# Other orders of work in an attention, Strassen feed-forward and Fourier kernel on one core

## The chip, the core and the metric

The kernel runs on one core of one Trainium2 chip. The metric is the device time of one execution in microseconds (us), as the median of several runs. A profile of one further execution stands beside them. Engines are called by the names of the profile: PE (TensorE, its weight loads apart as PEld), DVE (VectorE), ACT (ScalarE), POOL (GpSimd, called Pool in the text) and SP, which only issues transfers.

## The reference, cut to what matters

```python
x = windowed_attention(q, k, v)            # 2 batches, 8 heads, 768 x 64, ALiBi bias, 96 local keys and 8 global ones
x = x.transpose(0, 2, 1, 3).reshape(2, 768, 512)
u = x + (x.transpose(0, 2, 1) @ U @ V).transpose(0, 2, 1)        # rank 32
x = u + np.maximum(u @ w_ch1, 0) @ w_ch2                         # 512 -> 2048 -> 512
u = x + np.real(fft(fft(x, axis=1), axis=2))
un = (u - mean(u)) / np.sqrt(var(u) + 1e-6)
out = u + np.maximum(un @ moe2_w_ch1, 0) @ moe2_w_ch2
```

All is fp32. The kernel gets near full precision from PE by splitting each factor into a high part and the rest (names with H and L), and by three matmuls per product: high by high, high by low, low by high.

## The kernel before, in words

**Stages.** The attention is 48 steps of two query tiles each, run as slots 0 to 50 (a slot does the scores of its step, the transposes of the step two before, and the products with V of the step three before). Slots 0 to 32 (FFN_SLOT = 33) come first. Then come 32 rounds of the feed-forward part: rounds 0 to 7 are batch 0 of the first layer, 8 to 15 batch 1, 16 to 23 and 24 to 31 the second layer. The remaining 18 attention slots, the 22 mixing pieces of batch 1 (the rank 32 product), the splits of the next batch's factors and the Fourier steps are put between the items of the rounds.

**A round.** It makes 256 of the 2048 hidden columns, and adds their share of the output. The first product of the layer is done by the Winograd form of Strassen's scheme, in seven block products P1 to P7 (`product`, lines 706 to 735, six matmuls of 384 columns each). ITEMS (line 51) is the order of a round: P1, P5, L0, P6, L1, P2, L2, L3, P7, L4, L5, P3, P4. L0 to L5 are the six output tiles of the round before (`out_tile`, lines 737 to 756, six matmuls of 512 columns each). A gap is the place behind an item; gap number 13 g + i stands behind item i of round g, and `put` fills it (FILL, lines 314 to 317). All engines go through the items and gaps in the same order, each with its own part, in order.

**Banks.** P1 and P2 gather in Xb, P5 and P3 in Zb, P6, P7 and P4 in Yb. ACT copies P1 and P5 out (P1s, P5s), DVE adds P1s to Yb (L1262, item P6), ACT copies that back to P1s (L976), DVE adds it to Zb (L1266, item L1) and P5s to Yb into Xb (L1272, item P7). Four halves of the hidden block come from this; for each ACT does the relu (hidH, L962) and DVE the rest (hidL, L1242): relu(0, 0) at item P2, relu(1, 1) at P7, where it first waits until all tiles of the round before are made, relu(0, 1) at P3, relu(1, 0) at P4. The semaphore s_hidl counts the four. Each output tile takes one of two banks yP, and can start only when DVE has added the tile two before it to Y (L1249).

**Weights.** SP loads the first layer's blocks of a round two rounds ahead (w_load), and the output weights one round ahead (o_load). For round g + 1, ACT makes the high parts WCH in round g (`w_hi`, L952, part 0 at item L0 and part 1 at item L1; part 1 waits for the sums), and Pool the low parts WCL (`w_lo`, L518, four instructions). WOH is ACT's (L959, item L3), WOL Pool's (`o_lo`, L524, two instructions). `w_sums` (L507 to L512, Pool) makes the four sums of the weight blocks, two rounds ahead.

**The other factor.** RAW holds the transposed input of a batch, TT its four sums T1 to T4, made by `u_sums` on Pool (L542 to L548, 8 instructions over k = 0 to 3). UCH and UCL are the split factors. For batch 0 they are made in the attention (`first_split`, slots 15, 21, 27 and 32). For the others `split(c, name)` makes each of the seven in the gap 2, 4, 6, 7, 10, 13 or 15 places behind the start of the round before the change: ACT casts (L930) when the product that last used the old one is made, DVE subtracts (L1228). At the first, ACT waits for all the sums of that batch. CHANGES is 8, 16, 24. Pool's order in its loop (lines 550 to 575): w_lo(g + 1), o_lo(g), w_sums(g + 2), u_sums for a change at g + 2, then in rounds 7 and 8 the tables of the Fourier matrices, split into high and low (CSH, CSL: 2310 columns; CDH, CDL: 1028 columns). Ahead of the loop it is w_sums(0), w_lo(0), w_sums(1), u_sums(0, k).

**Fourier steps.** `fourier_slots` places them from round 8 (b + 1) + 1 on, for batch b. On DVE: fold (3 parts, twice), split, edge, seq, mid, and for each of three pairs of tiles dim (PE alone), combine (adds the transform to Y, then bn_stats and bn_aggr, L1346 to L1364), norm (L1374) and turn (PE transposes, ACT writes RAW, L1044). The first fold waits for CSL and CDL. Steps stand every 2.5 gaps per slot, at any item.

Of the kernel before, what the change touches and what calls it, by code (L numbers as in the profile page):

```python
# [22 lines left out]
ALU = mybir.AluOpType  # L23
# [27 lines left out]
ITEMS = ("P1", "P5", "L0", "P6", "L1", "P2", "L2", "L3", "P7", "L4", "L5", "P3", "P4")  # L51
PRODUCTS = ("P1", "P5", "P6", "P2", "P7", "P3", "P4")
# [45 lines left out]
def program(nc, q_t, k_t, v, k_win, v_win, n_local, n_global, moe_U, moe_V, w_in, w_out,  # L98
            seq_dft, dim_dft, ident_in, out):
    ctx = ExitStack()  # L100
    with ctx:
# [202 lines left out]
        FFN_SLOT = 33  # L304
# [31 lines left out]
        def split_slot(slot):  # L336

            return (slot - 15) // 6 if slot in (15, 21, 27) else KD - 1 if slot == FFN_SLOT - 1 else None
# [6 lines left out]
        for c, g in enumerate(CHANGES):  # L345
            for product, late in zip(PRODUCTS, (2, 4, 6, 7, 10, 13, 15)):
                put(GAPS * (g - 1) + late, "split", c, product)
# [25 lines left out]
        def fourier_slots(b):  # L373
            at = GAPS * (FPAIRS * (b + 1) + 1)

            def later(slot, *what):
                put(at + int(2.5 * slot), "fourier", b, *what)

            for slot, *what in ((0, "fold", 0, 0), (0.4, "fold", 0, 1), (0.8, "fold", 0, 2), (1.2, "split", 0), (2, "edge"), (4, "seq", 0, 0),
                                (4.4, "fold", 1, 0), (4.8, "fold", 1, 1), (5.2, "seq", 0, 1), (5.2, "fold", 1, 2), (7, "split", 1),  # L380
                                (9, "seq", 1, 0), (10, "seq", 1, 1), (11, "seq", 2, 0), (12, "mid")):
                later(slot, *what)
            order = []
            for i, slot in enumerate((13, 18, 22)):
                for part in range(2):
                    order.append((slot + part, 0, "dim", i, part))
                    for late, what in enumerate(("combine", "norm", "turn")):
                        order.append((16 + 4 * i + 2 * late + part, 1, what, i, part))
            for slot, _, *what in sorted(order, key=lambda o: o[:2]):
                later(slot, *what)  # L390
# [9 lines left out]
        def _(sp):  # L400
# [63 lines left out]
            for g in range(ROUNDS):  # L464
# [11 lines left out]
                if g == FPAIRS:  # L476
                    sp.wait_ge(s_csplit, 1)
# [13 lines left out]
        def _(pool):  # L491
# [60 lines left out]
            w_sums(1)  # L552
            for k in range(KD):
                u_sums(0, k)
            for g in range(ROUNDS):
# [3 lines left out]
                if g + 2 < ROUNDS:  # L559
                    w_sums(g + 2)  # L560
                if g + 2 in CHANGES:
                    for k in range(KD):
                        u_sums(CHANGES.index(g + 2) + 1, k)
# [900 lines left out]
```

## Time and profile before

| what | us |
|---|---|
| runs | 742.34, 742.73, 746.5 (median 742.73) |
| profiled execution | 743.1 |
| its span, first to last instruction | 741.3 |
| PE busy | 682.5 (92%), 3672 matmuls |
| PEld / DVE / ACT / POOL busy | 605.1 / 421.2 / 308.4 / 377.6 |
| mean granted clock of PE | 0.98 of full speed |

Busy time is that of one engine; engines overlap, so only the idle time of the engine that bounds a stage tells what can be won there. Idle time behind an item in brackets, as [2.65 <-DVE Y L1249], is the time the engine stood before this instruction, and what it waited for. Round g is counted from its first matmul of P1 to the next round's.

### The profile page before, as it was taken

What the parts mean: (1) busy time and instruction counts of PE and PEld (TensorE: products, weight loads), DVE (VectorE), ACT (ScalarE), POOL (GpSimd) and SP (SyncE); (2) the same over time, 40 slices, a digit from 0 to 9 for tenths busy, and PEclk for the clock granted to TensorE, in tenths of its full rate; (3) what the DMA queues carried; (4) which work ended last, traced back from release to release, by engine and by line L of the source; (5) the groups of instructions that cost most, each with busy time, mean ns of one, the idle gap of its engine ahead of it and who ended that gap; (6) DMA issues with size and microseconds to landing.
All of it is one profiled execution on the core that took longest, in us unless ns stands there. A gap on an engine that the chain in (4) does not pass through costs nothing.

```text
span 741.3 us, 10239 instructions
## 1 busy us (share of the span) xinstructions
PE 682.5 (92%) x3672; PEld 605.1 (82%) x3672; DVE 421.2 (57%) x903; ACT 308.4 (42%) x665; POOL 377.6 (51%) x365
## 2 busy tenths in 40 slices
PE   8949989999999988799997979999897889999997
PEld 6949889888898877688886869787786778899886
DVE  7526665544445386764675466653865485454544
ACT  4636676442433353234332444332343364334430
POOL 0140143244355899553453796555444876665621
PEclk9988999999999989999999999999999999999999
DMA  8332224012112313111110111111111022121132
GB/s 240 132 124 97 98 97 143 15 55 79 38 56 81 108 58 93 57 43 43 58 57 29 58 57 57 57 57 57 31 56 56 30 70 73 62 81 57 57 114 86
DMA packets 50532, 54.07 MB, mean 73 GB/s; under 512 B 4432, under 2 KB 37328, under 8 KB 50352
## 3 DMA queue, kind: packets, MB, share of 16 engines
q1 hardware_dynamic: 50480, 53.40, 22.9%
q8 instruction: 30, 0.49, 0.3%
q14 instruction: 22, 0.18, 0.1%
HBM read 53.39 MB, written 3.15 MB: 76 GB/s over the span
## 4 chain that ended last, share of the span: by engine, by line
PE 67%; DVE 12%; POOL 8%; ACT 6%; issue 5%; DMA 1%; DVEq 0%; SPq 0%; POOLq 0%; ACTq 0%
PE yP L753 10%; PE yP L755 9%; PE yP L754 9%; PE Yb L732 3%; PE Yb L733 3%; PE Yb L734 3%; PE aP L647 3%; PE aP L621 3%; PE Zb L732 2%; PE Zb L734 2%; PE Zb L733 2%; DVE Y L1249 2%; PE Xb L732 2%; PE Xb L733 2%; PE Xb L734 2%
## 5 line engine op out<-in xcount | busy, mean ns | idle before, releaser
L518 POOL TENSOR_TENSOR WCL<-w_stage,WCH 128x512 fp32r<-128x512 f32 (+1 forms) x128 | 154.7, 1230 | 204.9 <-ACT WCH L952 204.9
L1249 DVE TENSOR_TENSOR Y<-yP,Y 128x512 f32<-128x512 f32 x192 | 129.7, 684 | 89.4 <-PE yP L755 89.1
L753 PE MATMUL yP<-WOH,hidH 128*128 128x512 f32 x384 | 155.6, 405 | 24.6 <-DVE Y L1249 22.8
L755 PE MATMUL yP<-WOH,hidL 128*128 128x512 f32 x384 | 153.1, 399 | 0.0
L754 PE MATMUL yP<-WOL,hidH 128*128 128x512 f32 x384 | 152.6, 397 | 0.0
L524 POOL TENSOR_TENSOR WOL<-o_stage,WOH 128x512 fp32r<-128x512 f32 x64 | 86.0, 1366 | 46.6 <-ACT WOH L959 46.6
L753 PEld LDWEIGHTS yP<-WOH,hidH 128*128 128x128 f32 x384 | 73.5, 191 | 43.7 <-DVE Y L1249 28.2
L962 ACT ACTIVATE hidH<-Xb 128x384 fp32r<-128x384 f32 x64 | 31.4, 491 | 182.1 <-PE yP L755 174.3
L1242 DVE SCALAR_TENSOR_TENSOR hidL<-Xb,hidH 128x384 fp32r<-128x384 f32 x64 | 35.6, 556 | 89.8 <-ACT hidH L962 89.8
L755 PEld LDWEIGHTS yP<-WOH,hidL 128*128 128x128 f32 x384 | 73.0, 190 | 16.2
L754 PEld LDWEIGHTS yP<-WOL,hidH 128*128 128x128 f32 x384 | 73.3, 191 | 11.0
L732 PE MATMUL Yb<-UCH,WCH 128*128 128x384 f32 x192 | 66.5, 346 | 1.6 <-DVE UCL L1222 1.6
L733 PE MATMUL Yb<-UCL,WCH 128*128 128x384 f32 x192 | 65.5, 341 | 0.0
L734 PE MATMUL Yb<-UCH,WCL 128*128 128x384 f32 x192 | 65.4, 341 | 0.0
L952 ACT CAST WCH<-w_stage 128x768 fp32r<-128x768 f32 x64 | 60.2, 943 | 0.9 <-DMA w_stage<-w_in 0.9
L882 ACT ACTIVATE PB<-PB,nmax 128x232 f32<-128x232 f32 (+1 forms) x96 | 44.6, 465 | 30.2 <-DVE nmax L1169 29.9
L507 POOL TENSOR_TENSOR w_stage<-w_stage 128x256 f32<-128x256 f32 x32 | 24.0, 749 | 56.4 <-DMA w_stage<-w_in 56.4
L732 PE MATMUL Zb<-UCH,WCH 128*128 128x384 f32 x128 | 45.0, 352 | 4.2 <-DVE hidL L1242 4.2
L976 ACT COPY P1s<-Yb 128x384 f32<-128x384 f32 x32 | 15.4, 480 | 76.8 <-DVE Yb L1262 76.8
L732 PE MATMUL Xb<-UCH,WCH 128*128 128x384 f32 x128 | 43.6, 341 | 2.2 <-DVE hidL L1242 2.2
L647 PE MATMUL aP<-V,PT 128*128 128x64 f32 x264 | 34.9, 275 | 11.4 <-DVE PT L1177 9.5
L647 PEld LDWEIGHTS aP<-V,PT 128*128 128x128 f32 x264 | 33.2, 196 | 13.1 <-DVE PT L1177 10.1
(216 smaller groups left out, 1360.3 us busy)
## 6 DMA issues: line engine op xcount, KB each, us to landing
w_stage<-w_in SPq DMA_DIRECT2D x128, 128.0 KB, 2.3
o_stage<-w_out SPq DMA_DIRECT2D x32, 512.0 KB, 3.3
V<-v_win SPq DMA_DIRECT2D x8, 704.0 KB, 7.0
K<-k_win SPq DMA_DIRECT2D x8, 644.0 KB, 5.4
Q<-q_t SPq DMA_DIRECT2D x16, 192.0 KB, 3.4
Y<-x_scratch SPq DMA_DIRECT2D x8, 384.0 KB
out<-Y SPq DMA_DIRECT2D x12, 256.0 KB, 3.7
CSraw<-seq_dft SPq DMA_DIRECT2D x1, 1348.0 KB, 7.3
```

Of the source, the lines that this page charges most:

```text
L518: nc.gpsimd.tensor_tensor(WCL[:, g % 2, u0:u1, :, :], w_stage[:, 1 + u0:1 + u1, :, :], hi32(WCH[:, g % 2, u0:u1, :, :]), ALU.subtract).the ...
L524: nc.gpsimd.tensor_tensor(WOL[:, g % 2, f, :], o_stage[:, f, :], hi32(WOH[:, g % 2, f, :]), ALU.subtract).then_inc(s_ol, 1)
L647: mm = nc.tensor.matmul(OB[b][head % R][:, DH * t:DH * t + DH], PT[:, n % 2, P * x:P * x + P], V2[:, pair % 2, h, max(2 * t - 1, 0) + c, : ...
L732: nc.tensor.matmul(bank, wh, uh, start=first and k == 0, stop=False, skip_group_check=True)
L733: nc.tensor.matmul(bank, wh, ul, start=False, stop=False, skip_group_check=True)
L734: mm = nc.tensor.matmul(bank, wl, uh, start=False, stop=k == KF - 1, skip_group_check=True)
L753: nc.tensor.matmul(bank[:, :], hh, WOH[:, h % 2, f, :], start=f == 0, stop=False)
L754: nc.tensor.matmul(bank[:, :], hh, WOL[:, h % 2, f, :], start=False, stop=False)
L755: mm = nc.tensor.matmul(bank[:, :], hl, WOH[:, h % 2, f, :], start=False, stop=f == 1)
L882: nc.scalar.activation(PB[:, n % 3, i, 0:w], PB[:, n % 3, i, 0:w], ACT.Exp, bias=nmax[:, n % 3, i:i + 1], scale=-1.0, accum_out=psums[:, n ...
L952: nc.scalar.copy(WCH[:, g % 2, u, :, :], w_stage[:, u.start + 1:u.stop + 1, :, :]).then_inc(s_wh, 1)
L1249: nc.vector.tensor_tensor(y, yP[t % 2][:, :], y, ALU.add).then_inc(s_yadd, 1)
```

## The change

It changes orders alone; the arithmetic stays. The items P5 and P6 change places, and P3 and P4. Two more attention slots run ahead of the rounds (FFN_SLOT 35, the last first split at slot 33). The splits of a change stand at 3, 5, 7, 8, 15, 17 and 19, and ACT's wait there is one for RAW, and for the factor's own sums. All Fourier steps stand in gaps 1 to 8 of a round (CALM), one step number per gap, with the statistics as a step of their own. Pool does u_sums ahead of w_sums, in the loop and ahead of it, and its long table instructions in pieces. relu(1, 1) and its hidL step move from P7 and L4 to L5. Tile 0 waits for three of the four halves, tile 3 for the fourth.

```diff
-ITEMS = ("P1", "P5", "L0", "P6", "L1", "P2", "L2", "L3", "P7", "L4", "L5", "P3", "P4")
-PRODUCTS = ("P1", "P5", "P6", "P2", "P7", "P3", "P4")
+ITEMS = ("P1", "P6", "L0", "P5", "L1", "P2", "L2", "L3", "P7", "L4", "L5", "P4", "P3")
+PRODUCTS = ("P1", "P6", "P5", "P2", "P7", "P4", "P3")
+CALM = (1, 2, 3, 4, 5, 6, 7, 8)
...
-        FFN_SLOT = 33
+        FFN_SLOT = 35
...
-            return (slot - 15) // 6 if slot in (15, 21, 27) else KD - 1 if slot == FFN_SLOT - 1 else None
+            return (slot - 15) // 6 if slot in (15, 21, 27) else KD - 1 if slot == 33 else None
...
-            for product, late in zip(PRODUCTS, (2, 4, 6, 7, 10, 13, 15)):
+            for product, late in zip(PRODUCTS, (3, 5, 7, 8, GAPS + 2, GAPS + 4, GAPS + 6)):
                 put(GAPS * (g - 1) + late, "split", c, product)
...
-            at = GAPS * (FPAIRS * (b + 1) + 1)
-
-            def later(slot, *what):
-                put(at + int(2.5 * slot), "fourier", b, *what)
...
+            first = FPAIRS * (b + 1) + 1
+
+            def at(n, *what):
+                put(GAPS * (first + n // len(CALM)) + CALM[n % len(CALM)], "fourier", b, *what)
+
+            for n, *what in ((0, "fold", 0, 0), (1, "fold", 0, 1), (2, "fold", 0, 2), (3, "split", 0), (4, "edge"), (6, "seq", 0, 0),
+                             (7, "fold", 1, 0), (8, "seq", 0, 1), (8, "fold", 1, 1), (9, "fold", 1, 2), (10, "split", 1),
+                             (12, "seq", 1, 0), (13, "seq", 1, 1), (15, "seq", 2, 0), (16, "mid")):
+                at(n, *what)
+            for n in range(18, 42):
+                for i in range(HT):
+                    for late, *what in ((0, "dim", i, 0), (1, "dim", i, 1), (2, "combine", i, 0), (3, "stats", i, 0), (4, "combine", i, 1),
+                                        (5, "stats", i, 1), (6, "norm", i, 0), (7, "norm", i, 1), (7, "turn", i, 0), (8, "turn", i, 1)):
+                        if n == 18 + 7 * i + late:
+                            at(n, *what)
...
                 if g == FPAIRS:
-                    sp.wait_ge(s_csplit, 1)
+                    sp.wait_ge(s_csplit, 2 * HT)
...
             w_lo(0)
-            w_sums(1)
             for k in range(KD):
                 u_sums(0, k)
+            w_sums(1)
...
                 o_lo(g)
-                if g + 2 < ROUNDS:
-                    w_sums(g + 2)
                 if g + 2 in CHANGES:
                     for k in range(KD):
                         u_sums(CHANGES.index(g + 2) + 1, k)
+                if g + 2 < ROUNDS:
+                    w_sums(g + 2)
...
-                    nc.gpsimd.tensor_copy(CSH[:, :, :], CSdft).then_inc(s_csh, 1)
-                    pool.wait_ge(s_csh, 2)
-                    nc.gpsimd.tensor_tensor(CSL[:, :, :], CSdft, hi32(CSH[:, :, :]), ALU.subtract).then_inc(s_csplit, 1)
+                    for t in range(HT):
+                        nc.gpsimd.tensor_copy(CSH[:, t, :], CSdft[:, t, :]).then_inc(s_csh, 1)
+                    pool.wait_ge(s_csh, 1 + HT)
+                    for t in range(HT):
+                        for c in (slice(0, CN), slice(CN, CN + HALF)):
+                            nc.gpsimd.tensor_tensor(CSL[:, t, c], CSdft[:, t, c], hi32(CSH[:, t, c]), ALU.subtract).then_inc(s_csplit, 1)
...
-                    nc.gpsimd.tensor_tensor(CDL[:, :, :], CDraw, hi32(CDH[:, :, :]), ALU.subtract).then_inc(s_csplit, 1)
+                    for k in range(KF):
+                        nc.gpsimd.tensor_tensor(CDL[:, k, :], CDraw[:, k, :], hi32(CDH[:, k, :]), ALU.subtract).then_inc(s_csplit, 1)
...
-                        pe.wait_ge(s_hidl, 4 * (g - 1) + {"P1": 2, "P5": 3, "P6": 4}[name])
+                        pe.wait_ge(s_hidl, 4 * (g - 1) + {"P1": 2, "P6": 3, "P5": 4}[name])
...
-                if t == 0:
-                    pe.wait_ge(s_hidl, 4 * (h + 1))
+                if t % HT == 0:
+                    pe.wait_ge(s_hidl, 4 * h + (3 if t == 0 else 4))
...
-                if j == 0:
-                    act.wait_ge(s_tadd, 2 * KD * (c + 2))
+                if j == 0 and c == 0:
+                    act.wait_ge(s_raw, 2 * PAIRS)
+                elif j == 0:
+                    act.wait_ge(s_unr, NT * c)
+                if op >= T1:
+                    act.wait_ge(s_tadd, 2 * KD * (c + 1) + {T1: 2, T2: 6, T4: 7, T3: 8}[op])
...
-                elif item == "P7":
+                elif item == "L5":
                     act.wait_ge(s_x22, g + 1)
...
-                elif item == "L4":
+                elif item == "L5":
                     lo(g, 2, 1, 1, Xb)
+                elif item == "P4":
+                    lo(g, 3, 1, 0, Yb)
                 elif item == "P3":
-                    lo(g, 3, 0, 1, Zb)
-                elif item == "P4":
-                    lo(g, 4, 1, 0, Yb)
+                    lo(g, 4, 0, 1, Zb)
...
+                elif what == "stats":
+                    i, part = at
+                    n = HT * b + i
+                    y = Y[:, base + HT * part + i, :]
                     dve.wait_ge(s_u2, 2 * (2 * n + part) + 2)
                     nc.vector.bn_stats(stat[:, part, :], y).then_inc(s_st, 1)
```

## Rows read from the trace of the kernel before

**Rows 1.** The page, busy time by engine
```profile
PE 682.5 (92%) x3672; PEld 605.1 (82%) x3672; DVE 421.2 (57%) x903; ACT 308.4 (42%) x665; POOL 377.6 (51%) x365
```

**Rows 2.** Stretches: length, busy PE, PEld, DVE, ACT, POOL, PEclk, DMA, GB/s
```profile
0.00:97.00 97.00, 80.95 (x574) 75.06 (x574) 54.50 (x209) 55.92 (x183) 18.90 (x27) 0.95 0.42 132
96.97:250.92 153.95, 147.77 (x865) 134.76 (x865) 79.56 (x190) 69.17 (x163) 69.12 (x71) 1.00 0.25 81
250.92:272.28 21.36, 18.71 (x79) 16.34 (x79) 12.00 (x18) 9.57 (x15) 19.73 (x17) 0.84 0.13 38
272.28:292.88 20.60, 17.70 (x79) 15.31 (x79) 15.72 (x17) 7.39 (x12) 20.22 (x15) 0.92 0.31 96
292.88:316.99 24.11, 20.07 (x91) 17.02 (x91) 15.09 (x30) 7.68 (x16) 13.81 (x13) 0.93 0.15 44
316.99:421.99 105.00, 98.98 (x506) 85.59 (x506) 63.22 (x126) 38.58 (x70) 51.06 (x51) 0.98 0.16 51
421.99:458.72 36.73, 32.17 (x158) 27.93 (x157) 22.88 (x34) 17.07 (x27) 31.76 (x28) 1.00 0.19 58
458.72:582.15 123.43, 115.90 (x595) 100.03 (x595) 77.10 (x155) 44.95 (x85) 62.02 (x62) 1.00 0.17 52
...
681.43:697.07 15.64, 15.64 (x80) 14.09 (x80) 7.61 (x14) 6.03 (x10) 9.90 (x10) 1.00 0.22 68
```

**Rows 3.** The gap in the head: Pool's timeline, PE's wait, the stretch of low clock
```profile
41.03 4.41 POOL L518 TENSOR_TENSOR WCL<-w_stage,WCH 128x512 fp32r<-128x512 f32 x4 [16.87 <-ACT WCH L952]
...
52.49 0.99 POOL L542 TENSOR_TENSOR TT<-RAW 128x384 f32<-128x384 f32 x1
...
PE aP L647 <- DVE PT L1177: 9.5, 1, 9.5
...
49.78:60.02 10.24, 3.64 (x16) 3.59 (x17) 4.11 (x15) 3.61 (x12) 3.63 (x5) 0.50 0.00 0
```

**Rows 4.** ACT's timeline in round 1, and PE's waits from 136 to 200 us
```profile
142.40 0.49 ACT L962 ACTIVATE hidH<-Xb 128x384 fp32r<-128x384 f32 x1 [5.23 <-PE yP L755]
...
PE aP L634 <- ACT PT L891: 1.4, 1, 1.4
```

**Rows 5.** Timelines of Pool, ACT and PE at the first change
```profile
247.90 0.75 POOL L507 TENSOR_TENSOR w_stage<-w_stage 128x256 f32<-128x256 f32 x1
...
257.88 1.02 POOL L548 TENSOR_TENSOR TT<-RAW 128x384 f32<-128x384 f32 x1
...
258.99 0.83 ACT L930 CAST UCH<-RAW 128x768 fp32r<-128x768 f32 x1 [4.58 <-POOL TT L548]
...
262.07 0.79 PE L753 MATMUL yP<-WOH,hidH 128*128 128x512 f32 x1 [2.65 <-DVE Y L1249]
```

**Rows 6.** Timelines of Pool and DVE around the tables, and line L1228
```profile
245.40 2.55 POOL L524 TENSOR_TENSOR WOL<-o_stage,WOH 128x512 fp32r<-128x512 f32 x2 [0.68 <-ACT WOH L959]
...
266.17 3.97 POOL L524 TENSOR_TENSOR WOL<-o_stage,WOH 128x512 fp32r<-128x512 f32 x2
...
276.24 5.76 POOL L569 TENSOR_TENSOR CSL<-CSraw,CSH 128x2310 fp32r<-128x2310 f32 x1
...
277.49 5.32 DVE L1228 TENSOR_TENSOR UCL<-TT,UCH 128x768 fp32r<-128x768 f32 x1
...
296.63 1.64 DVE L1296 TENSOR_TENSOR EO<-Y 128x384 f32<-128x384 f32 x1 [2.47 <-POOL CDL L575]
...
L1228 DVE TENSOR_TENSOR UCL<-TT,UCH x12: 960/1332/5324, 263.6 to 607.5; 128x768 fp32r<-128x768 f32 x12
```

**Rows 7.** Two lines of combine (min/median/max ns), PE's waits 520 to 570 and at the end
```profile
L1356 DVE TENSOR_TENSOR Y<-Y,DIF x6: 428/429/1556, 363.2 to 560.8; 128x257 f32<-128x257 f32 x6
...
L1359 DVE BATCH_NORM_STATS2 stat<-Y x12: 693/694/696, 365.7 to 564.9; 128x6 f32<-128x512 f32 x12
...
PE Zb L732 <- DVE hidL L1242: 1.5, 1, 1.5
...
PE yP L753 <- DVE hidL L1242: 1.2, 1, 1.2
```

More of the change, by code:

```diff
@@ L373, in fourier_slots @@
         def fourier_slots(b):
-            at = GAPS * (FPAIRS * (b + 1) + 1)
-            def later(slot, *what):
-                put(at + int(2.5 * slot), "fourier", b, *what)
[L379 to L390, printed above, removed]
+            first = FPAIRS * (b + 1) + 1
[11 more added lines that the diff above has]
+                            at(n, *what)
         for b in range(B):
@@ L573, in _ @@
                     nc.gpsimd.tensor_copy(CDH[:, :, :], CDraw).then_inc(s_csh, 1)
-                    pool.wait_ge(s_csh, 4)
-                    nc.gpsimd.tensor_tensor(CDL[:, :, :], CDraw, hi32(CDH[:, :, :]), ALU.subtract).then_inc(s_csplit, 1)
+                    pool.wait_ge(s_csh, HT + 3)
+                    for k in range(KF):
+                        nc.gpsimd.tensor_tensor(CDL[:, k, :], CDraw[:, k, :], hi32(CDH[:, k, :]), ALU.subtract).then_inc(s_csplit, 1)
         @block.tensor
@@ L764, in fourier @@
                     if n == 0:
-                        pe.wait_ge(s_csplit, 2)
+                        pe.wait_ge(s_csplit, 2 * HT + KF)
                     if m == KF:
@@ L1260, in item_done @@
                     dve.wait_ge(s_p1s, g + 1)
-                    dve.wait_ge(s_prod, len(PRODUCTS) * g + 3)
+                    dve.wait_ge(s_prod, len(PRODUCTS) * g + 2)
                     nc.vector.tensor_tensor(Yb[:, 0:BLK], Yb[:, 0:BLK], P1s[:, :], ALU.add).then_inc(s_y16, 1)
@@ L1293, in fourier @@
                         if m == 0:
-                            dve.wait_ge(s_csplit, 2)
+                            dve.wait_ge(s_csplit, 2 * HT + KF)
                             dve.wait_ge(s_yadd, TILES_OUT * FPAIRS * (b + 1))
```

## The prediction

> **What bounds the kernel now.** I read the page's busy shares, then one table of stretches, then the timelines around each gap of TensorE. PE is busy 92% of the span [rows 1], so what can be won is its idle time, and the time in which it runs at the lower of its two clock levels. A round of the feed-forward part with nothing in its gaps takes 15.64 us and leaves PE no gap (last row of [rows 2]). Against that, in the same table, duration minus PE busy is idle time, and what remains after idle time and 15.64 us per round is clock loss or extra PE work: round 7: 2.65 idle and 3.07 more at clock 0.84; round 8: 2.90 and 2.06; round 9: 4.04 and, with its Fourier matmuls, 4.43; rounds 10 to 14: 6.02; 15 and 16: 4.56 (23 and 24 repeat it); 17 to 22: 7.53. Rounds 0 to 6 have 6.18, the stage ahead of them 97.00 - 80.95 = 16.05, of which one gap is 9.5 [rows 3]. The reader sees a kernel bound by PE, in which two dozen gaps, all at changes of stage, cost some 50 us together with the clock.
>
> **The change, part by part.** All sums are made against the profiled execution, 743.1 us (span 741.3 and 1.8 around it); the median of the runs is 742.73, 0.4 lower.
>
> (a) Pool's u_sums(0) ahead of w_sums(1). In [rows 3] Pool ends w_lo(0) at 41.03 + 4.41 = 45.44, then stands before w_sums(1), which waits for its weights; only at 52.49 comes L542, for which ACT, behind it DVE and behind DVE PE (9.5) wait. Its input is ready, so L542 starts at 45.44: 7.05 earlier, and the gap shrinks to about 2.4. w_sums(1) now comes after u_sums(0, 3), a few us before ACT wants it in round 0; its cover is those products. From 49.78 to 60.02 the clock was at its lower level, with PE busy 3.64 [rows 3]: between 0 and 1.8 comes back, I take 0.5. **-7.6** (-6.5 to -9).
>
> (b) FFN_SLOT 35, the last split at slot 33. Two attention slots move from rounds where PE is 96% busy (147.77 of 153.95) to a stage where it is 83% (80.95 of 97.00). Rounds 0 to 6 hold 153.95 - 7 x 15.64 = 44 us or more of 18 slots and 22 mixing pieces, so a slot is 1 to 2.5 us of PE; two of 2 us cost 4 x (1/0.83 - 1/0.96) = 0.65 more. P6 is now second and needs all splits, with one slot and one product ahead of it where it had two products and one slot; in return no bias copies stand before the split on ACT. **+0.5** (-1.6 to +2.5).
>
> (c) relu(1,1) behind the last tile. ACT issued it at P7, where it sat 5.23 us for the tiles [rows 4], with the exponentials and RAW copies of the fills behind it, for which PE then waited 1.4 [rows 4]; with two like it this is some 3.2 of the 6.18 us of rounds 0 to 6 [rows 2]. At L5 the wait is nearly over when ACT comes. The next product into that bank is P1, two products later; relu 0.49 and the DVE step 0.56 behind the evacuation of the last tile fit with some 0.6 to spare. **-2.5** (0 to -4).
>
> (d) Rounds 7 to 9. Before, the split of P1's factor waited for all sums: Pool ends L548 at 258.90, ACT starts at 258.99 after 4.58 idle, and tile 2 waited on PE until 262.07 [rows 5]. Now the sums start at 247.90 instead of 250.82, factors made of RAW don't wait for them, and the first split stands one item later. But w_sums(8) ends only where the sums ended, at 258.9, and ACT's w_hi(8, 1) (item L1, wanted 5.1 us into the round, at 256.0) needs it. ACT stands 2.9 us, relu of P2, DVE's step on it and tile 2's evacuation behind it; with the splits in the way PE loses about 2.0 at L4 and 0.9 at the next P1, where it lost 2.65. The gain is rather in round 8: CSL was one instruction of 5.76 us, and a DVE split that began 1.25 into it took 5.32 where its least is 0.96 [rows 6]; with pieces of about 1 us a DVE step waits 1 at most, and most of round 8's 2.90 goes, and the clock with it. What is late next is Pool: from 247.90 to the end of CDL at 296.6 it worked nearly without a pause, and only idle and stretch of 2 to 3 us can go (WOL took 3.97 for two where 2.55 is usual [rows 6]). CDL then ends near 294. Round 9 would start at 250.92 + 2 x 15.64 + 2.9 = 285.1; the first fold stands behind P6, at 287.8, and DVE is held there 6 us (2.47 before, [rows 6]) with the evacuations queued behind it. Tile 2 can't start at 291.9, but near 296, and the fold steps cost 1.5 more: 5.5 idle. Round 10 starts at 285.1 + 15.64 + 2.4 of Fourier matmuls + 5.5 = 308.6 instead of 316.99, -8.4. Gaps of 5.5 bring a stretch of low clock again, +2. **-6.5** (0 to -14).
>
> The Trainium skill (SBUF — State Buffer, section "SBUF: two separate sides") says that VectorE with two SBUF inputs and GpSimd hold a shared port pair as an exclusive lock for a whole instruction. The 5.32 beside the 5.76 agrees with it. By that rule each end of a short Pool piece also lets a waiting DVE step in, and Pool, which is late here, ends later for it; what that gives is the first rival.
>
> (e) The changes at 16 and 24 are the same without CSL: 4.56 idle in two rounds [rows 2], twice; by the working of (d) 2.9 stays and 0.4 of a split in the next round goes. The late splits are spread over items L0, L1, L2 of the next round, free of cost beside 15.6 us of products. **-4** for both (0 to -8).
>
> (f) Fourier steps in gaps 1 to 8 alone. Before, combine, stats and norm fell into any gap: one combine with statistics is 0.43 x 4 + 0.69 + 0.18 on DVE, one took 1.56 for one of these [rows 7], and when it falls beside the last items, the hidL steps behind it are late for the next products (1.5 [rows 7]). Now stats (0.69 [rows 7]) are a step of their own and none stands where relu, hidL and the next product follow each other. The folds of batch 1 still crowd into items 1 to 5 of round 17 (about 1.5 of idle stays), and each of six combines, up to 1.7 us ahead of an evacuation with 1.5 to 2.4 us of room, may cost 0.3 to 0.6. Rounds 10 to 14: 6.02 and 1.7 of clock become 2: -5.7. Rounds 17 to 22: 7.53 becomes 3.5: -4. **-9.7** (0 to -14).
>
> (g) P4 ahead of P3, and tile 0 waiting for three halves, not four. In steady rounds P6 takes Yb 2.05 after P4's end, and relu and DVE need 1.3: nothing changes. After the last round tile 0 waited 1.2 for Yb's half [rows 7]; P3 (1.03) now hides that. **-1.0**.
>
> Sum: -7.6 + 0.5 - 2.5 - 6.5 - 4 - 9.7 - 1.0 = -30.8: 712.3 for the profiled execution, 712 for the median.
>
> **Rivals.**
> 1. Pool stays the bound of rounds 7 to 9. For it: Pool has some 46 us of work there against 47 of PE; the stretched WOL. Eight short pieces that each let a DVE step of 0.96 in put CDL up to 7 us later, at 296 to 301; then nothing is won in (d): 712 + 6.5 = 718.5, 720 with more low clock. Against: DVE has few such steps there.
> 2. The wait for w_sums takes the whole place of the wait for u_sums: (e) gives nothing, 716.
> 3. More goes than I count: w_sums is done early enough, combines fit, the low clock doesn't come back. Another 4 in (d), 4 in (e), 3 in (f): 701.
> 4. The other side: dense Fourier steps. DVE does 33 steps per batch, 66 in all, now in 40 neighbouring gaps each; if each delays an evacuation on which PE waits, the time is 712 + 9.7 - 15.3 (the old waits and clock) + 66c. It passes 743 when c is over 0.55 us. At 0.65 it is 749. For it: the single gaps in [rows 2] come from such steps. Against: they cost 13.55 / 66 = 0.2 each today, in worse places. A half of it, c = 0.35, gives 729.
> 5. The order doesn't do what it says in the head: Pool finds another wait and (a) halves: 716.
>
> **How the numbers follow.** Forecast (708 to 716) 0.50; more gone (701) 0.18; Pool (719) 0.15; rivals 2 and 5 (716) 0.07; rival 4 at half price (729) 0.07, at full price (749) 0.03. All bounds on the good side give 691, all on the bad side 741. The range 701 to 727 leaves out about 0.2. A difference under 1%, 7.4 us, is what a measurement hardly tells from none; faster by more (below 735.3): 0.94, within: 0.03, slower: 0.03.
>
> **What would show each step.** (a): L542 right after the first four L518, PE's gap in the head under 3 us. (b): P6 of round 0 waits 1 to 2 us for UCL. (c): no wait of PE for PT or RAW in rounds 1 to 4. (d), (e): ACT idle before the second WCH cast with L512 as its releaser; CSL in six pieces of about 1 us and no DVE step over 2.5; a wait of DVE for CDL of 5 us or more before the first fold; round 10 near 8 us earlier relative to round 7. (f): idle of rounds 17 to 22 near 3.5. (g): no wait before the last tile 0. I am wrong if round 9 has no gap (then the time is lower), or if rounds 10 to 14 and 17 to 22 keep theirs.

## The result, and the profile after

The changed kernel takes **749.98 us** (median of 8 runs, 748.53 to 754.58), the kernel before 742.84 (8 runs): a ratio of 1.0098, 95% interval [1.0069, 1.0126]. It is 1% slower where 712 was predicted, outside the range 701 to 727 and on the other side of no change. The profiled execution took 751.75 us, its span is 750.0, with a mean granted clock of 0.968, where it was 0.982.

The page's busy line of the changed kernel, against [rows 1]:

```profile
PE 696.1 (93%) x3672; PEld 612.6 (82%) x3672; DVE 438.2 (58%) x903; ACT 309.8 (41%) x665; POOL 382.3 (51%) x373
```

The matmuls are as many as before, but PE is busy 13.6 us longer, and DVE 17.0 with the same 903 instructions. So the same work runs slower on two engines: PE, for the most part, at its lower clock level, DVE in stretched instructions. Where that is shows in the stretches, with the columns of [rows 2]: the head, rounds 0 to 6, 7, 8, 9, 10 to 14, 15 and 16, 17 to 22, and one round of the end with nothing in its gaps.

```profile
0.00:92.73 92.73, 86.07 (x604) 79.13 (x604) 56.07 (x216) 59.97 (x193) 18.92 (x27) 0.98 0.45 142
92.73:238.90 146.17, 143.31 (x836) 130.97 (x835) 77.70 (x182) 65.22 (x152) 69.30 (x69) 1.00 0.26 82
238.90:258.82 19.92, 17.49 (x80) 15.18 (x79) 13.91 (x18) 8.96 (x14) 19.65 (x18) 0.91 0.17 53
258.82:275.00 16.18, 16.07 (x80) 13.84 (x79) 12.15 (x17) 8.14 (x13) 16.09 (x16) 1.00 0.21 62
275.00:301.96 26.96, 20.38 (x91) 16.59 (x90) 17.12 (x32) 7.81 (x16) 20.41 (x20) 0.94 0.21 67
301.96:422.29 120.33, 106.82 (x505) 90.07 (x505) 67.63 (x124) 39.08 (x70) 51.48 (x49) 0.91 0.15 44
422.29:457.82 35.53, 33.10 (x158) 29.36 (x157) 25.33 (x34) 17.09 (x27) 31.13 (x28) 0.95 0.18 52
457.82:593.04 135.22, 121.69 (x594) 102.87 (x594) 84.26 (x155) 45.45 (x85) 64.31 (x61) 0.96 0.17 49
691.12:706.71 15.59, 15.59 (x79) 14.06 (x79) 7.61 (x14) 6.03 (x10) 9.63 (x10) 1.00 0.23 65
```

Length by stage, this table less [rows 2] (the predicted column is by the prediction's terms):

| stage | before | after | difference | predicted |
|---|---|---|---|---|
| head, rounds 0 to 6: (a), (b), (c) | 250.92 | 238.90 | -12.0 | -9.6 |
| rounds 7 and 8 | 41.96 | 36.10 | -5.9 | } -6.5 |
| round 9 | 24.11 | 26.96 | +2.9 | } |
| rounds 10 to 14 | 105.00 | 120.33 | **+15.3** | -5.7 |
| rounds 17 to 22 | 123.43 | 135.22 | **+11.8** | -4.0 |
| rounds 15, 16 and 23, 24 | 73.45 | 71.05 | -2.4 | -4.0 |
| rounds 25 to 31 and the end | 122.43 | 121.44 | -1.0 | -1.0 |

All of the loss, 27.1 us, lies in the two stretches with the Fourier steps. The rest won 18.4, where 21.1 was predicted. Both sides of the table are single executions. The two Fourier stretches of the kernel before repeat to 0.1 us (105.03 and 123.51 in g3 below, whose code there is the same), but its rounds 7 and 8 don't: the same code took 36.73 us in g3 and 36.70 in e2, not 41.96. PE's waits in rounds 17 to 22 of the changed kernel (total, times, longest):

```profile
PE aP L830 <- DVE UN L1385: 5.5, 2, 4.8
PE yP L756 <- DVE Y L1256: 5.0, 5, 1.9
PE aP L782 <- DVE EOL L1322: 2.3, 1, 2.3
```

None of the three is the wait for hidL that the prediction watched: PE waits for DVE's norm, for its evacuations and for a fold's split. DVE's timeline in round 13, from combine to norm (start, length):

```profile
389.21 1.51 DVE L1364 TENSOR_TENSOR Y<-Y,SUM 128x255 f32<-128x255 f32 x1
390.64 0.68 DVE L1256 TENSOR_TENSOR Y<-yP,Y 128x512 f32<-128x512 f32 x1
...
392.95 1.32 DVE L1363 TENSOR_TENSOR Y<-Y,SUM 128x257 f32<-128x257 f32 x1
394.19 1.48 DVE L1364 TENSOR_TENSOR Y<-Y,DIF 128x255 f32<-128x255 f32 x1
395.59 0.68 DVE L1256 TENSOR_TENSOR Y<-yP,Y 128x512 f32<-128x512 f32 x1
...
397.12 0.52 DVE L1375 TENSOR_SCALAR rstd<-mv 128x2 f32<-128x2 f32 x1
...
398.34 0.55 DVE L1385 TENSOR_SCALAR UN<-Y,mv,rstd 128x512 f32<-128x512 f32 x1
```

and beside it Pool's and PE's:

```profile
389.06 2.79 POOL L517 TENSOR_TENSOR WCL<-w_stage,WCH 128x512 fp32r<-128x512 f32 x2 [2.77 <-ACT WCH L959]
392.69 2.70 POOL L523 TENSOR_TENSOR WOL<-o_stage,WOH 128x512 fp32r<-128x512 f32 x2 [0.84 <-ACT WOH L966]
...
398.94 1.11 PE L830 MATMUL aP<-identf,UN 128*128 128x128 f32 x4 [4.81 <-DVE UN L1385]
```

The reader sees additions of 255 and 257 columns that take 1.3 to 1.5 us beside WCL or WOL, where their least is 0.41 and 0.43, an evacuation out of a bank of PE (L1256, 390.64) that keeps its 0.68 beside the same WCL, and at the end PE standing 4.81 us at a turn, which is all that its order has next. From 396.2 on the clock was at its lower level for 6.8 us. Line L1364 over the whole run (least, median, longest, in ns):

```profile
L1364 DVE TENSOR_TENSOR Y<-Y,SUM x6: 408/1484/1510, 345.0 to 560.3; 128x255 f32<-128x255 f32 x6
L1364 DVE TENSOR_TENSOR Y<-Y,DIF x6: 410/1478/1507, 350.8 to 565.2; 128x255 f32<-128x255 f32 x6
```

and the same line of the kernel before:

```profile
L1357 DVE TENSOR_TENSOR Y<-Y,SUM x6: 416/420/951, 364.7 to 561.2; 128x255 f32<-128x255 f32 x6
```

The Trainium skill (SBUF — State Buffer, section "SBUF: two separate sides") gives the shape of it: VectorE with two SBUF inputs and GpSimd exclude each other for a whole instruction, so a step that meets one waits its rest out. The trace agrees, the unstretched L1256 with its PSUM input included; the prediction used the rule for the tables and didn't apply it to the combines.

### The profile page after: what moved, and what is told of

Read it like the earlier page. It is cut to its first block, busy times and chain, and to the rows that moved or that the text cites. A ratio compares the mean times of both kernels' runs of the same rounds, so it can differ in the third digit from the quotient of the medians.

```text
span 750.0 us, 10293 instructions
## 1 busy us (share of the span) xinstructions
PE 696.1 (93%) x3672; PEld 612.6 (82%) x3672; DVE 438.2 (58%) x903; ACT 309.8 (41%) x665; POOL 382.3 (51%) x373
## 4 chain that ended last, share of the span: by engine, by line
PE 63%; DVE 14%; POOL 12%; issue 5%; ACT 4%; DMA 1%; SPq 0%; DVEq 0%; ACTq 0%; POOLq 0%
PE yP L756 8%; PE yP L758 8%; PE yP L757 8%; POOL WCL L517 4%; PE Yb L735 3%; PE Yb L737 3%; PE Yb L736 3%; PE aP L624 3%; PE aP L650 2%; PE Xb L735 2%; PE Zb L735 2%; PE Zb L737 2%; PE Zb L736 2%; PE Xb L736 2%; PE Xb L737 2%
## 5 line engine op out<-in xcount | busy, mean ns | idle before, releaser
L517 POOL TENSOR_TENSOR WCL<-w_stage,WCH 128x512 fp32r<-128x512 f32 (+1 forms) x128 | 154.1, 1229 | 207.0 <-ACT WCH L959 207.0
L1256 DVE TENSOR_TENSOR Y<-yP,Y 128x512 f32<-128x512 f32 x192 | 129.5, 685 | 105.7 <-PE yP L758 105.0
L756 PE MATMUL yP<-WOH,hidH 128*128 128x512 f32 x384 | 159.0, 414 | 22.6 <-DVE Y L1256 22.2
L758 PE MATMUL yP<-WOH,hidL 128*128 128x512 f32 x384 | 156.3, 407 | 0.0
L757 PE MATMUL yP<-WOL,hidH 128*128 128x512 f32 x384 | 155.5, 405 | 0.0
L758 PEld LDWEIGHTS yP<-WOH,hidL 128*128 128x128 f32 x384 | 74.8, 195 | 17.0
L757 PEld LDWEIGHTS yP<-WOL,hidH 128*128 128x128 f32 x384 | 75.1, 196 | 11.8
L736 PE MATMUL Zb<-UCL,WCH 128*128 128x384 f32 x128 | 43.4, 339 | 0.0
L737 PE MATMUL Zb<-UCH,WCL 128*128 128x384 f32 x128 | 43.3, 339 | 0.0
L736 PE MATMUL Xb<-UCL,WCH 128*128 128x384 f32 x128 | 43.0, 336 | 0.0
L737 PE MATMUL Xb<-UCH,WCL 128*128 128x384 f32 x128 | 42.9, 335 | 0.0
```

The source lines that it names most:

```text
L517: nc.gpsimd.tensor_tensor(WCL[:, g % 2, u0:u1, :, :], w_stage[:, 1 + u0:1 + u1, :, :], hi32(WCH[:, g % 2, u0:u1, :, :]), ALU.subtract).the ...
L736: nc.tensor.matmul(bank, wh, ul, start=False, stop=False, skip_group_check=True)
L737: mm = nc.tensor.matmul(bank, wl, uh, start=False, stop=k == KF - 1, skip_group_check=True)
L756: nc.tensor.matmul(bank[:, :], hh, WOH[:, h % 2, f, :], start=f == 0, stop=False)
L757: nc.tensor.matmul(bank[:, :], hh, WOL[:, h % 2, f, :], start=False, stop=False)
L758: mm = nc.tensor.matmul(bank[:, :], hl, WOH[:, h % 2, f, :], start=False, stop=f == 1)
```

## The experiments

**1. The places alone, both ways.** e1 is the changed kernel with the old places; e2 the old kernel with nothing of the change but the new ones.

e1, on the changed kernel:

```diff
-            for n, *what in ((0, "fold", 0, 0), ...
+            for slot, *what in ((0, "fold", 0, 0), (0.4, "fold", 0, 1), ...
+                later(slot, *what)
...
+                if what[0] == "combine":
+                    later(slot, "stats", *what[1:])
```

e2, on the kernel before:

```diff
-                put(at + int(2.5 * slot), "fourier", b, *what)
+                put(GAPS * (first + n // len(CALM)) + CALM[n % len(CALM)], "fourier", b, *what)
...
+                elif what == "stats":
```

> The changed kernel with the Fourier steps at their places of before (every 2.5 gaps per slot, statistics directly behind the combine), all else as changed. Rounds 10 to 14 lost 15 us and rounds 17 to 22 lost 12 us in the changed kernel against before; rounds 0 to 8 had won 18. Theory 'places' (the new places of the Fourier steps cost it, whatever the reason): these 27 us come back, rounds 17 to 22 take 119 to 124 us, and the time is 719 to 725 us. Rival 'orders' (the new order of the products and the relu behind L5 harm the Fourier rounds): the rounds stay slow, 740 to 750 us.

> The kernel before with the new places of the Fourier steps alone (statistics as a step of their own). Theory 'places': rounds 10 to 14 and 17 to 22 get slower by some 27 us together, round 9 about as before: 765 to 772 us. Rival 'orders': within 5 us of before, 738 to 748 us.

e1: **721.81 us**, ratio 0.9729 [0.9682, 0.9776]. e2: **767.32 us**, 1.0329 [1.0291, 1.0366]. The new places cost 28.2 us on top of the change (749.98 - 721.81) and 23.9 on the kernel before (767.32 - 743.42): the same edit, with and without all others. Rounds 17 to 22 of e1, then of e2:

```profile
441.46:562.20 120.74, 115.39 (x595) 100.12 (x594) 80.11 (x155) 45.03 (x85) 63.40 (x61) 1.00 0.18 55
```

```profile
467.00:601.93 134.93, 121.70 (x594) 103.36 (x594) 83.05 (x155) 44.90 (x85) 63.24 (x62) 0.96 0.16 47
```

e2's row is the changed kernel's but for 0.3 us. So the failed step is (f), and it needs none of the other edits. In rounds 10 to 14 and 17 to 22 together the places cost 23.7 us in e2 (117.18 + 134.93, less 228.43) and 33.9 against e1 (100.91 and 120.74); the other edits had won 6.8 there, which leaves the 27.1.

**2. Pool or crowding.** e3 leaves Pool's WCL and WOL nearly out in the rounds with Fourier steps; e4 keeps Pool's work and gives each step 1.75 gaps in place of one, at any item; f1 does both.

e3 on the changed kernel, and f1 on e4 (the same is done to WOL):

```diff
+LIGHT = tuple(range(9, 15)) + tuple(range(17, 23))
...
-                    nc.gpsimd.tensor_tensor(WCL[:, g % 2, u0:u1, :, :], w_stage[:, 1 + u0:1 + u1, :, :], hi32(WCH[:, g % 2, u0:u1, :, :]), ALU.subtract).then_inc(s_wl, 1)
+                    (nc.gpsimd.tensor_tensor(WCL[:, g % 2, u0:u1, :, :], w_stage[:, 1 + u0:1 + u1, :, :], hi32(WCH[:, g % 2, u0:u1, :, :]), ALU.subtract) if g - 1 not in LIGHT else nc.gpsimd.tensor_tensor(WCL[:, g % 2, u0:u0 + 1, 0, 0:2], w_stage[:, 1 + u0:2 + u0, 0, 0:2], hi32(WCH[:, g % 2, u0:u0 + 1, 0, 0:2]), ALU.subtract)).then_inc(s_wl, 1)
```

e4, on the changed kernel:

```diff
-                put(GAPS * (first + n // len(CALM)) + CALM[n % len(CALM)], "fourier", b, *what)
+                put(GAPS * first + int(1.75 * n), "fourier", b, *what)
```

> The changed kernel in which Pool makes only two columns of each piece of WCL and WOL in rounds 9 to 14 and 17 to 22, so the low parts of the weights are old ones there; the places of all steps stay. Theory 'shared port' (DVE's Fourier steps are stretched because Pool is at work in just these gaps): DVE busy of rounds 17 to 22 falls from 84.3 to 78 us or less, most of the idle time goes, and rounds 17 to 22 fall from 135.2 to 122 to 126 us, the time to 722 to 732. Rival 'crowding' (one step per gap ahead of the evacuations is too much, with Pool or without): DVE busy falls but idle and low clock stay, rounds 17 to 22 stay above 130 us, the time above 740.

> The changed kernel with the same list of Fourier steps spread evenly over all 13 gaps, one every 1.75 gaps, with the same first and nearly the same last gap. 'Crowding': rounds 17 to 22 fall to 120 to 125 us, the time to 722 to 730. 'Shared port' alone: about half of the steps still lie beside Pool's work, rounds 17 to 22 near 129, the time near 736.

> The spread placement with Pool's WCL and WOL cut to two columns in rounds 9 to 14 and 17 to 22 (old low parts of the weights there). It is the fourth corner beside the changed kernel (rounds 17 to 22 in 135.2 us), the changed kernel with light Pool (126.2) and spread with full Pool (119.0). If the port costs only in gaps 1 to 8: 117 to 119 us, so that of the 16 us between calm and spread 9 are Pool's and 7 crowding. If light Pool helps everywhere alike, by some 9: 110 us; but 115.9 is the PE work, so that can't be, and the idle time left is at most 3.1.

One run each: e3 727.36, e4 716.9, f1 706.96. Rounds 17 to 22 of e3, of e4 and of f1:

```profile
444.06:570.24 126.18, 119.21 (x594) 101.86 (x594) 73.93 (x155) 45.51 (x85) 28.50 (x64) 0.97 0.17 53
```

```profile
438.85:557.84 118.99, 115.87 (x594) 99.96 (x594) 79.75 (x155) 45.18 (x85) 64.52 (x61) 1.00 0.18 55
```

```profile
433.18:550.08 116.90, 115.39 (x595) 100.18 (x594) 73.56 (x155) 45.21 (x85) 27.41 (x63) 1.00 0.19 57
```

| | rounds 17 to 22: Pool full / light | rounds 10 to 14: Pool full / light |
|---|---|---|
| gaps 1 to 8 only | 135.2 / 126.2 | 120.3 / 110.0 |
| 1.75 gaps a step | 119.0 / 116.9 | 100.8 / 99.2 |

WCL and WOL cost 9.0 and 10.3 us where the steps are dense, 2.1 and 1.6 where they are spread. With them nearly out, the dense places still cost 9.3 and 10.9; Pool's w_sums remain there (it is busy 28.5 of the 126.2 us). Both causes are real: taken out in this order, the 18.3 us between the corners of the first column are 9.0 for WCL and WOL and 9.3 for the dense places, and spreading alone removes 16.2. The single runs are firm by stage: five later kernels with e4's places (f2, f4, f5, g2, g4) have 100.7 to 100.8 and 119.0 again. f1 is 9.9 us below e4 as a whole, but only 3.7 of it lies in these two stretches. "Dense" stands for two things at once, one step per gap and the gaps 1 to 8 with their four tiles; spreading changed both, and neither was tried apart. What is left in e3 and shrinks in e4, in PE's waits of rounds 17 to 22 (e3, then e4):

```profile
PE aP L831 <- DVE UN L1386: 3.6, 2, 2.8
PE yP L757 <- DVE Y L1257: 1.3, 3, 0.9
```

```profile
PE aP L830 <- DVE UN L1385: 1.0, 2, 0.6
PE yP L756 <- DVE Y L1256: 0.9, 1, 0.9
```

In the changed kernel and in e3 the turn stands one gap behind the norm it needs. Which of the two it is, that distance or DVE's queue in general, wasn't tried apart.

**3. Round 9: the fold's wait.** In the changed kernel the first fold waits for CDL, since EO lies in the place of the table's raw copy. f2 (on e4) lays EO and MIR behind EOH and EOL; the fold then needs CSL only, and the split of it waits for CDL.

```diff
-            EO = sb("EO", [P, 2, HT, P], F32, f)
-            MIR = sb("MIR", [P, 2, HT, P], F32, f)
             EOH = sb("EOH", [P, 2, HT, P], F32R, f)
             EOL = sb("EOL", [P, 2, HT, P], F32R, f)
+            EO = sb("EO", [P, 2, HT, P], F32, f)
+            MIR = sb("MIR", [P, 2, HT, P], F32, f)
...
+                    else:
+                        act.wait_ge(s_csplit, 2 * HT + KF)
...
-                            dve.wait_ge(s_csplit, 2 * HT + KF)
+                            dve.wait_ge(s_csplit, 2 * HT)
...
+                    if n == 0:
+                        dve.wait_ge(s_csplit, 2 * HT + KF)
```

> Spread placement, and the buffers EO and MIR of the fold laid beside the part of CSraw that holds the second table, so that the first fold waits for CSL only and EOH, EOL wait for CDL. Theory (the wait of DVE for CDL in round 9 costs PE some 5 to 7 us, low clock included): round 9 falls from 26.5 to 19 to 21 us, the time to 710 to 712. Rival (the fold's own work ahead of the evacuations costs it, or the split then waits as long): round 9 stays over 24 us, the time 715 to 717.

714.86 us, ratio 0.9606 [0.9559, 0.9654]; round 9 takes 23.3 us, e4's 26.5. DVE's wait for CDL (8.1 us in e4) is gone, and a wait for the split that now stands behind CDL is in its place; of e4:

```profile
DVE EO L1303 <- POOL CDL L578: 8.1, 1, 8.1
```

and of f2:

```profile
DVE F0L L1325 <- ACT EOH L1018: 2.1, 1, 2.1
```

Taking the fold off that wait was worth 3.2 us, less than expected (19 to 21 us for the round, 710 to 712 in all), since the split still needs CDL, and CDL itself came later: 47.5 us behind the start of round 7, where it was 45.3 in e4.

**4. Tables whole again.** f4 is e4 with CSH, CSL and CDL as one instruction each.

> Spread placement with Pool's table instructions whole, as before the change. Theory of the prediction (a DVE split behind a whole CSL stands 5 us and costs round 8 its gap of 2.9 and a low clock): rounds 7 and 8, 36.1 us with pieces, take 38 to 41 us. Rival (the splits stand elsewhere now and hardly meet CSL): under 37 us.

718.33 us (one run): rounds 7 and 8 take 38.2 (e4: 36.1), round 9 24.3 (26.5). Pool's CSL and the split beside it in f4:

```profile
264.25 5.19 POOL L568 TENSOR_TENSOR CSL<-CSraw,CSH 128x2310 fp32r<-128x2310 f32 x1
...
265.73 4.53 DVE L1231 TENSOR_TENSOR UCL<-TT,UCH 128x768 fp32r<-128x768 f32 x1 [0.57 <-ACT UCH L933]
```

and CSL in pieces, in e4:

```profile
262.91 7.35 POOL L571 TENSOR_TENSOR CSL<-CSraw,CSH 128x386 fp32r<-128x386 f32 x6
```

Pieces spare round 8 a DVE step of 4.5 us and make CSL 2.2 us longer. The WCL behind it gives part of that back (5.21 us for 6.62), so that CDL ends 1.0 later (45.3 us behind the start of round 7, 44.3 in f4). Round 9 is shorter in f4 mainly because it starts 2.1 us later and meets the same CDL. The sum of rounds 7 to 9 is the same to 0.1 us (62.5 and 62.6). Whole tables together with f2's layout weren't tried.

**5. Order on Pool at the changes.** f5 is e4 with w_sums ahead of u_sums, as before; g2 is f2 with ACT's w_hi(g + 1, 1) three items later (L3) in the rounds ahead of a change.

f5:

```diff
+                if g + 2 < ROUNDS:
+                    w_sums(g + 2)
                 if g + 2 in CHANGES:
...
-                if g + 2 < ROUNDS:
-                    w_sums(g + 2)
```

g2:

```diff
-                elif item == "L1" and g + 1 < ROUNDS:
+                elif item == ("L3" if g + 1 in CHANGES else "L1") and g + 1 < ROUNDS:
                     w_hi(g + 1, 1)
-                elif item == "L3":
+                if item == "L3":
```

> Spread placement with w_sums ahead of u_sums again in the loop. Theory (the wait for w_sums took the place of the wait for u_sums, price for price): rounds 7, 15 and 23 stay within 1 us of 19.9, 20.4 and 20.1. If the order was worth what the prediction gave it, they get 1 to 2 us slower each; if the late w_sums is the worse of the two, they get faster.

> Spread placement, fold free of CDL, and ACT's w_hi(g + 1, 1) behind L3 instead of L1 in the rounds ahead of a change, so that it doesn't stand for w_sums there. Theory (ACT's wait for w_sums is what makes the gap of 2.6 to 3.1 in these rounds): rounds 7, 15 and 23 fall from 19.9, 20.4 and 21.7 to 16 to 18 us each, the time to 705 to 708. Rival (Pool is late anyway and now P1 of the next round waits for WCL): rounds 7, 15, 23 save it, the gap stands ahead of rounds 8, 16 and 24 and the time stays above 711.

f5 712.85, g2 707.43 (one run each). f5's rounds 15 and 16 take 33.4 us (e4: 36.0), 23 and 24 33.3 (35.9): u_sums first costs 2.6 us at each of these, where the expectation was no difference. At the first change round 7 gains as much (17.3 for 19.9), and round 8 loses it again, 18.8 against 16.2. PE's wait there in f5:

```profile
PE Xb L735 <- POOL WCL L517: 2.9, 1, 2.9
```

What u_sums first costs is ACT's wait for w_sums with the splits behind it; of the changed kernel, 238 to 260 us:

```profile
ACT WCH L959 <- POOL w_stage L511: 2.8, 1, 2.8
```

g2 takes it away without touching Pool's order: rounds 15 and 23 take 17.7 each (e4: 20.4, 20.1). At the first change it moves the loss and wins nothing, as the rival said: round 7 takes 17.3 and round 8 19.2, together 36.4 (36.1).

**6. relu(1, 1) back at P7.** g1 is e4 with ACT's relu at P7 and DVE's step at L4.

```diff
-                elif item == "L5":
+                elif item == "P7":
                     act.wait_ge(s_x22, g + 1)
...
-                elif item == "L5":
+                elif item == "L4":
                     lo(g, 2, 1, 1, Xb)
```

> Spread placement with relu(1, 1) at P7 and its hidL step at L4 again. Theory of the prediction (ACT stands at P7 for the tiles, with the fills behind it): rounds 0 to 6, 146.3 us with the relu behind L5, take 149 to 151; the Fourier rounds 17 to 22, 119.0, lose 1 to 3 more, since their ACT steps stand in the same gaps; time 720 to 724. Rival (the gaps of PE in rounds 0 to 6 went for another reason, the places of the fills): within 1 us of 716.9.

732.48 us, ratio 0.9861 [0.9834, 0.9889], against e4's one run of 716.9, where 720 to 724 was expected: with these places the move is worth 14.4 us by stages; the head, which it doesn't touch, holds 1.1 of the 15.5 between the spans. By stages, g1 less e4: rounds 0 to 6 +2.7, round 7 +2.0, round 8 -0.2, round 9 -1.8, 10 to 14 +3.9, 15 and 16 +2.2, 17 to 22 +4.0, 23 and 24 +1.6. ACT's timeline of g1 at round 8:

```profile
261.28 0.49 ACT L969 ACTIVATE hidH<-Xb 128x384 fp32r<-128x384 f32 x1 [5.47 <-PE yP L758]
261.67 0.83 ACT L937 CAST UCH<-RAW 128x768 fp32r<-128x768 f32 x1
```

ACT stands 5.47 us in front of a tile with the next split queued behind. In the Fourier rounds ACT's copies and casts are queued behind it in the same way (at 530.57 relu after 4.44 us of standing, then the copy Qs, for which DVE had waited 2.98), and PE waits for what follows them (448 to 572 us):

```profile
PE Xb L735 <- DVE hidL L1249: 2.3, 2, 1.5
PE Yb L735 <- DVE hidL L1249: 1.9, 2, 1.4
```

**7. The head alone.** g3 is the kernel before with u_sums(0, k) ahead of w_sums(1), nothing else.

> The kernel before with u_sums(0) ahead of w_sums(1) in the head and nothing else. Theory of the prediction: the 9.5 us gap shrinks to about 2.5, the low clock stretch of 10.2 us to 3.4 or none, round 0 begins at 89 to 90 us instead of 97.0, and the time is 734 to 736 us. Rival (w_sums(1), now late, holds round 0 or 1 up): 738 or more.

735.11 us, ratio 0.9894 [0.9867, 0.9921]: -7.2, with round 0 starting at 89.64 instead of 96.97. Its gap in the head, where [rows 3] had 9.5:

```profile
PE aP L647 <- DVE PT L1177: 2.4, 1, 2.4
```

**8. The version that comes out of it.** g4 is f2 with w_sums first at the changes at 16 and 24, and u_sums first with the late w_hi at 8.

```diff
+                if g + 2 < ROUNDS and g + 2 != FPAIRS:
+                    w_sums(g + 2)
                 if g + 2 in CHANGES: ...
-                if g + 2 < ROUNDS:
+                if g + 2 == FPAIRS:
                     w_sums(g + 2)
...
-                elif item == ("L3" if g + 1 in CHANGES else "L1") and g + 1 < ROUNDS:
+                elif item == ("L3" if g + 1 == FPAIRS else "L1") and g + 1 < ROUNDS:
                     w_hi(g + 1, 1)
-                elif item == "L3":
+                if item == "L3":
```

> Spread placement, fold free of CDL, w_sums ahead of u_sums at the changes 16 and 24 (no tables there), u_sums first at change 8 with w_hi(8, 1) behind L3. Expected from the runs so far: rounds 15 and 23 at 17.6, round 7 at 16 to 18, round 9 at 23.3: 706 to 709 us. If the cover of these gaps was common (one low clock stretch less moves the others), 711 or more.

**707.69 us, ratio 0.9526 [0.95, 0.9552]** against the kernel before, 4.7% faster, and 42 us faster than the changed kernel. It isn't told from g2's one run of 707.43. Its busy line, and its rounds 7 and 8, 9, 15 and 16, 17 to 22:

```profile
PE 675.4 (96%) x3672; PEld 600.2 (85%) x3672; DVE 425.7 (60%) x903; ACT 309.5 (44%) x665; POOL 385.6 (55%) x373
```

```profile
241.24:277.67 36.43, 32.04 (x157) 27.88 (x157) 26.16 (x37) 17.57 (x28) 36.09 (x34) 1.00 0.19 57
277.67:298.86 21.19, 19.86 (x89) 17.46 (x90) 13.86 (x27) 7.41 (x15) 20.95 (x20) 0.92 0.25 73
399.63:432.92 33.29, 31.75 (x157) 28.08 (x157) 24.03 (x34) 17.08 (x27) 31.54 (x28) 1.00 0.19 60
432.92:551.91 118.99, 115.84 (x594) 99.93 (x594) 79.73 (x155) 45.18 (x85) 64.43 (x62) 1.00 0.18 55
```

PE is busy 20.7 us less than in the changed kernel with the same matmuls, and most of that is the clock: PE is busy 6.8 us at the lower level here and 44.0 in the changed kernel, and half of the 37.1 between them is 18.6, as an estimate.

## Why the prediction was wrong

**(f), the step that failed** ("Fourier steps in gaps 1 to 8 alone", -9.7): measured +27.1. It looked at one chain, relu, hidL and the next product, and gaps 1 to 8 are indeed clear of that. It didn't ask what else is in those gaps. Pool's WCL and WOL of each round are (384.3 to 395.4 us in the round shown), and four of the tiles with their evacuations. So a step moved off the hidL chain moved onto Pool and onto the evacuations. It then priced a combine by the unstretched rows ("0.43 x 4"), though the 1.56 stood beside it in [rows 7] as the case that happened "for one of these"; in the new places the longer one is the median of L1364. The mechanism was written down as rival 4, "dense Fourier steps", with 749 at c = 0.65 and a chance of 0.03. From -15.3 + 66c = 27.1 the measured c is 0.64. Against it the prediction held that the steps "cost 13.55 / 66 = 0.2 each today, in worse places". That was the error: the price before the change was one of spread steps, with 2.5 gaps to a slot, and says nothing on dense ones. The range of (f) ended at 0 all the same, though rival 4 puts it at +28, so the stated bad side (741, where its bounds add up to 738) couldn't hold what came. With 1.75 gaps per step the two stretches gain 8.6 (4.2 and 4.4, e4 against [rows 2]), near the 9.7 forecast; 6.8 of that e1 has with the old places.

**(a)**, -7.6: shown, -7.3 in g3. In the changed kernel L541 starts right behind the four L517, as was said, at 45.58, and PE's wait for PT is 0.7.

**(b)**, +0.5: the head is 3.1 longer than g3's (two slots more), rounds 0 to 6 5.0 shorter (g1, with relu at its old place, against g3: 148.95 and 153.99). That makes -1.9; but round 0's start scatters by 3.3 us among the eleven kernels with the same head (92.53 in f1 to 95.80 in e1), and with their mean of 94.2 it is -0.5. Its size is small, its sign open, and 1.4 of the 12.0 won ahead of round 7 is luck of this kind. P6 of round 0 waits 1.4 for UCL, as foretold.

**(c)**, -2.5: in rounds 0 to 6 g1 shows 2.7. But the move was costed there alone. At the changes and among the Fourier steps, ACT's splits and casts stood behind the same wait, and over the whole kernel it is worth 14.4. It is the largest edit on the good side, and what (f) was to win comes from it: with relu at P7 the spread places took 0.2 and 0.5 off the two Fourier stretches (g1: 104.76 and 122.95), with relu at L5 4.2 and 4.4 (e4).

**(d)**, -6.5: measured -3.0 (round 7's start to round 10's, 66.07 and 63.06), and not even that is shown to be (d)'s. Rounds 7 and 8, then round 9, of g3 and of e2, whose code there is the old one but for e2's Fourier places in round 9:

```profile
243.63:280.36 36.73, 33.59 (x158) 29.11 (x158) 23.19 (x34) 17.07 (x27) 34.98 (x26) 0.95 0.19 57
280.36:309.94 29.58, 21.94 (x91) 18.11 (x91) 15.06 (x30) 7.68 (x16) 18.84 (x19) 0.83 0.19 59
```

```profile
250.52:287.22 36.70, 33.56 (x158) 29.13 (x157) 23.21 (x34) 17.09 (x27) 34.95 (x26) 0.95 0.19 58
287.22:313.09 25.87, 20.35 (x90) 16.53 (x90) 16.97 (x32) 7.69 (x16) 20.21 (x19) 0.93 0.23 67
```

g3 takes 66.3 like the kernel before, though none of its splits is longer than 1.53 us: the split of 5.32 in [rows 6] belongs to one execution, and what it cost rounds 7 and 8 there, round 9 costs in g3. e2 takes 62.6 with the new places alone, 3.5 less than the kernel before, and e1 63.7 with all but the new places, 2.3 less; together they give the 3.0, so beside the new places the edits of (d) win nothing. What failed in (d) is the end of CDL, set at "near 294", which is 43.1 behind the start of round 7. CDL in the kernel before, then in the changed one:

```profile
294.19 2.41 POOL L575 TENSOR_TENSOR CDL<-CSraw,CDH 128x1028 fp32r<-128x1028 f32 x1
```

```profile
281.75 2.51 POOL L578 TENSOR_TENSOR CDL<-CSraw,CDH 128x514 fp32r<-128x514 f32 x2
```

It ends 45.7 and 45.4 behind that start (45.6 in g3 and e2). Pool's chain to CDL stayed the bound, as rival 1 had it: it reached CSH 2.1 us earlier than before, and the pieces of CSL (7.35 us, 5.76 before and 5.19 in f4 in one) gave most of it back. Rounds 7 and 8 were to take 34.2 and take 36.1; the 1.9 are in round 7, where the wait of ACT came as foretold but brought a stretch of lower clock at 252.9 that had not been counted. Round 9 was to take 23.5 and 2 of clock, and takes 26.96: DVE was held 6.24 us for CDL (6 foretold), PE stood 6.6 (5.5), and clock cost 20.38 - 15.64 - 2.4 = 2.3. The wait came out near 6 because the round and CDL were both some 2 us later than forecast.

**(e)**, -4: measured -2.4; idle time fell by 4.3, near the forecast, and 1.9 came back as PE time at the lower clock (33.1 busy for 32.2, twice). With w_sums first and spread places it is -6.8 (f5: 33.4 and 33.3 for 36.73). "2.9 stays", ACT's wait for w_sums, was right in size, and it is the price of the new order on Pool.

**(g)**, -1.0: measured -0.94 behind the last round, and nothing waits ahead of the last tile 0.

## What to carry to other kernels

A gap is quiet only if all engines' work in it is looked at: before moving VectorE steps with two SBUF inputs, lay GpSimd's timeline of one period over the new places, and price each step by the stretched duration if they meet. The cost of a spread step doesn't price the same step packed one per gap; spread the steps as far as the stage allows, and leave more than one gap between a step and the TensorE step that needs it (likely, though the distance wasn't tried apart here). Before a gap is priced from one trace, look at the same stage in a second execution: the longest VectorE step of rounds 7 to 9 was there in one and gone in two others, g3 and e2. A wait for the newest result on an in-order engine costs whatever is queued behind it in every stage, so price such a move once per stage, the special ones first.

## What the runs showed of the hardware that was not expected

- A 255-column addition on VectorE with both inputs in SBUF had a median of 1.48 us beside Pool's subtractions, and 0.42 with these nearly left out (e3, medians of 419 and 418 ns). Additions with one input in a bank of PE (L1256) took 0.66 to 0.69, all 192 of them.
- Pool's 5.19 us subtraction, cut into six (f4 whole, e4 in pieces), took 7.35 us in all. Three splits of DVE, of 1.5 to 1.7 us each, ran within that time; that the 2.2 us are theirs is likely and wasn't tried apart.
- Gaps of PE of 1.95 to 2.43 us (ahead of 435.7, 488.7 and 521.2) had a stretch of 3.4 us at the lower clock level at or right behind them. Of two gaps of 4.81, the one ahead of 398.9 had a stretch of 6.8 and the one ahead of 570.0 one of 3.4, and in the kernel before the gap of 2.65 ahead of 433.1 had none. So equal gaps don't cost the same clock. The changed kernel has 12 such stretches, 47.8 us with PE busy for 44.0, against 5, 27.3 and 20.0 before; half of the difference in busy time, 12.0, is an estimate of the clock's part in the 13.6 us that PE is busier.
